# Two fused feed-forward layers on one core: every product and transpose cut to 64 rows, top and low half of the array as two streams

## The reference, cut to what matters

```
x   : 4 x 4096 x 192;  weight : 8 heads x 7 taps, softmaxed over the taps
a   = sum over k of w[head, k] * x[position - 6 + k]          (each head has 24 of the 192 columns)
h1  = a @ moe_w_in          (192 x 2048);   g1 = h1 * cos(h1)
y1  = g1 @ moe_w_out        (2048 x 192)
h2  = y1 @ moe2_w_in        (192 x 2048);   g2 = max(h2, 0)^2
out = g2 @ moe2_w_out       (2048 x 192)
```

## Time and profile before

| what | value |
|---|---|
| median of 3 runs | 2475.63 us (2473.64 to 2476.59) |
| the profiled execution's own time | 2478.0 us |
| its span | 2476.2 us |
| TensorE busy | 2409.9 us, 97% of the span, 10880 products and transposes |
| VectorE, ScalarE busy | 1869.2 us (75%), 1738.2 us (70%) |
| mean granted TensorE clock | 0.993 of full speed |
| transfers | 32.89 MB, 13 GB/s over the span |

### The profile page before, as it was taken

The page is one execution under the profiler, slowest core; times in us unless marked ns, Lnnn a source line. Parts: engine busy times, 40 slices in busy tenths (PEclk is TensorE's granted clock), DMA queues, the critical chain, the costliest instruction groups (busy, mean ns, idle before and its releaser), DMA issues.

```text
span 2476.2 us, 29392 instructions
## 1 busy us (share of the span) xinstructions
PE 2409.9 (97%) x10880; PEld 1994.4 (81%) x10880; DVE 1869.2 (75%) x2061; ACT 1738.2 (70%) x1805; POOL 24.8 (1%) x11
## 2 busy tenths in 40 slices
PE   4699999999999999999999999999999999999998
PEld 3488888888888888888888888888888888888886
DVE  7787777777777777777777777778777778777752
ACT  4577677767677767777767777776777776777774
POOL 1200000000000000000000000000000000000000
PEclk9899999999999999999999999999999999999998
DMA  3100000000000000000000000000000000000000
GB/s 108 39 1 13 14 9 10 13 6 13 13 6 13 13 6 13 13 6 13 8 11 13 13 6 13 6 13 13 13 6 13 6 13 13 13 6 6 7 7 13
DMA packets 39456, 32.89 MB, mean 13 GB/s; under 512 B 1676, under 2 KB 38668, under 8 KB 39180
## 3 DMA queue, kind: packets, MB, share of 16 engines
q1 hardware_dynamic: 39260, 32.61, 4.4%
q10 hardware_dynamic: 176, 0.00, 0.0%
HBM read 20.03 MB, written 12.58 MB: 13 GB/s over the span
## 4 chain that ended last, share of the span: by engine, by line
PE 94%; DVE 3%; ACT 2%; DMA 0%; issue 0%; SPq 0%; ACTq 0%
PE h L320 9%; PE h L321 9%; PE h L323 9%; PE h L322 9%; PE h L324 9%; PE y_B L340 5%; PE y_A L340 5%; PE y_B L341 5%; PE y_B L344 5%; PE y_B L342 5%; PE y_B L343 5%; PE y_A L342 5%; PE y_A L341 5%; PE y_A L343 5%; PE y_A L344 5%; PE h L366 1%
## 5 line engine op out<-in xcount | busy, mean ns | idle before, releaser
L554 DVE TENSOR_TENSOR g_lo<-g,g_hi 128x1024 fp32r<-128x1024 f32 x512 | 629.8, 1230 | 280.3 <-ACT g_hi L456 278.4
L456 ACT ACTIVATE g_hi<-g 128x1024 fp32r<-128x1024 f32 x512 | 538.0, 1051 | 50.0 <-DVE g L549 49.6
L446 ACT ACTIVATE w<-w,quarter 128x1024 f32<-128x1024 f32 x256 | 295.2, 1153 | 373.3 <-DVE w L542 373.3
L436 ACT ACTIVATE g<-h 128x1024 f32<-128x1024 f32 x256 | 261.2, 1020 | 199.6 <-PE h L324 199.5
L549 DVE TENSOR_TENSOR g<-w,g 128x1024 f32<-128x1024 f32 x256 | 316.0, 1234 | 60.1 <-ACT w L446 41.4
L542 DVE SCALAR_TENSOR_TENSOR w<-w,g 128x1024 f32<-128x1024 f32 x256 | 313.7, 1225 | 8.8
L540 DVE TENSOR_SCALAR w<-g 128x1024 f32<-128x1024 f32 x256 | 179.2, 700 | 147.8 <-ACT g L436 147.7
L438 ACT ACTIVATE g<-h 128x1024 f32<-128x1024 f32 x256 | 260.1, 1016 | 43.5 <-PE h L324 41.0
L440 ACT ACTIVATE g<-g 128x1024 f32<-128x1024 f32 x256 | 271.9, 1062 | 8.1
L340 PE MATMUL y_A<-g_hi,dn_lo_A 128*128 128x512 f32 x512 | 207.1, 405 | 24.4 <-DVE g_lo L554 24.4
L320 PE MATMUL h<-x_side_A,up_side_lo_A 128*128 128x512 f32 x512 | 200.5, 392 | 24.4 <-DVE x_side_A L589 20.5
(11 more groups left out here) (90 smaller groups left out, 4254.7 us busy)
## 6 DMA issues: line engine op xcount, KB each, us to landing
rows_in<-x SPq DMA_DIRECT2D x32, 384.0 KB, 3.3
out<-late SPq DMA_DIRECT2D x32, 384.0 KB, 2.6
late<-w_out SPq DMA_DIRECT2D x2, 1536.0 KB, 10.8
g<-w_in SPq DMA_DIRECT2D x1, 1024.0 KB, 5.7
g<-w_in SPq DMA_DIRECT2D x2, 512.0 KB, 8.6
late<-w_in SPq DMA_DIRECT2D x2, 512.0 KB, 4.4
late<-w_in SPq DMA_DIRECT2D x4, 256.0 KB, 5.5
taps<-weight ACTq DMA_DIRECT2D x4, 0.7 KB
```

What stands on the lines that cost most here:

```text
L446: act.activation(v, v, ACT.Sin, bias=quarter[:, 0:1], scale=-TURN).then_inc(cosine, 1)
L456: act.activation(g_hi[:, r, :, :], g[:, r, :, :], ACT.Copy).then_inc(hi_made[kind], 1)
L554: dve.tensor_tensor(g_lo[:, r, :, :], g[:, r, :, :], g_hi[:, r, :, :].bitcast(F32), ALU.subtract).then_inc(lo_made[kind], 1)
```

## The change

The array of 128 rows is used as two halves. Every product takes 64 rows of the stationary and of the moving operand: rows 0 to 63 (`top`) or 64 to 127 (`low`). TensorE's instructions alternate between the halves. In `up_and_down` the top half does the up projection of the slot (9 steps) and then its share of the down projection (10 steps), while the low half does the down projection first (10) and the up projection after it (9): 19 steps of one product on each half. Both halves add into the same bank, one after the other, and new semaphores (`up_top`, `down_top`, `down_low`, `turned_low`) keep them from being in one bank at once.

The side's low-by-high product needs 64 rows only. So an up projection has 4.5 products of 128 rows for a chunk in place of 5: 9 steps a half for the pair. For the odd chunk this needs the side's high part in the other 64 rows as well (`x_odd`), for the even chunk the weights (`up_even`); the copies to `x_odd` are one more ScalarE instruction for each tile of layer 1 and one more VectorE instruction for layer 2.

`LAG` becomes 4. Where the down projection's slot is X or Y there is none to pair with, and two up projections are joined with one down projection (`two_up_and_down`, 28 steps). X and Y slots pair transposes with a down projection (`turn_and_down`, 14 steps); a transpose is now of 64 rows, with a weight load of 128 columns and 64 moving columns, so there are twice as many. B0 moves from slot 2 to slot 3, and the splits of y_A and y_B move one slot later on ScalarE and VectorE. The halves of the output's side are added by ScalarE and VectorE (`y2_low`, `y2_summed`) where a product with the matrix `fold` did it.

```diff
-LAG = 3
-SLOTS = [("A", 0), ("A", 1), ("B", 0), ("A", 2), ("X", 0), ("B", 1), ("A", 3), ("B", 2), ("A", 4),
+LAG = 4
+SLOTS = [("A", 0), ("A", 1), ("A", 2), ("B", 0), ("X", 0), ("B", 1), ("A", 3), ("B", 2), ("A", 4),
          ("B", 3), ("A", 5), ("Y", 0), ("A", 6), ("B", 4), ("A", 7), ("B", 5), ("B", 6), ("B", 7)]
...
-            def up(turn, s, kind, p):
+
+
+            UP, DOWN = 4 * PAIR + 1, 5 * PAIR
+            SHORT = 2 * CB
+
+            def up_waits(turn, s, kind, p):
+                freed = turn.before(turn.slots, s, HB)
+                if freed:
+                    pe.wait_ge(taken[freed[0]], freed[1])
...
+                    pe.wait_ge(even_made, 2)
+
+            def up_step(turn, s, kind, p, rows, k):
+
+                even = 5 if rows is hi_rows[kind] else 4
+                n, j = (0, k) if k < even else (1, k - even)
+                if rows is low and j == 0:
+                    pe.wait_ge(up_top[kind][n], turn.count(kind, p))
+                f = slice((p * PAIR + n) * P, (p * PAIR + n + 1) * P)
+                dst = h[:, s % HB, n, :]
+                end = k in (even - 1, UP - 1)
+                z = rows is low and end
+                if j == 0:
+                    mm = pe.matmul(dst, up_side[kind][rows, f], xin_side[kind][rows, :], start=rows is top, stop=z)
+                if j == 1:
+                    mm = pe.matmul(dst, up_lo[kind][rows, f], xin_hi[kind][rows, :], start=False, stop=z)
+                if j == 2:
+                    mm = pe.matmul(dst, up_hi[kind][rows, f], xin_lo[kind][rows, :], start=False, stop=z)
+                if j == 3:
+                    mm = pe.matmul(dst, up_hi[kind][rows, f], xin_hi[kind][rows, :], start=False, stop=z)
+                if j == 4 and n == 0:
+                    mm = pe.matmul(dst, up_even[rows, p, :], xin_side[kind][rows, :], start=False, stop=z)
+                if j == 4 and n == 1:
+                    mm = pe.matmul(dst, up_side[kind][rows, f], xin_odd[rows, :], start=False, stop=z)
+                if rows is top and end:
+                    mm.then_inc(up_top[kind][n], 1)
+                if rows is low and k == UP - 1:
+                    mm.then_inc(filled[kind], 1)
+
...
                 if kind == "B" and p == 0 and turn.runs("Y"):
                     pe.wait_ge(y2_copied, turn.i - 1)
+                    pe.wait_ge(y2_summed, turn.i - 1)
                 pe.wait_ge(lo_made[kind], turn.count(kind, p, back))
+
+            def down_step(turn, r, kind, p, back, rows, k, first):
+
+                if k in (0, 6):
+                    other = (down_low if rows is top else down_top)[kind][k // 6]
+                    n = turn.count(kind, p, back) - (rows is first)
+                    if not isinstance(n, int) or n > 0:
+                        pe.wait_ge(other, n)
...
+                if m == 0 and j == 0:
+                    mm = pe.matmul(y[kind][:, 0, :], dn_lo[kind][rows, c, :], hi, start=a, stop=False)
...
+                if k in (5, DOWN - 1):
+                    mm.then_inc((down_top if rows is top else down_low)[kind][m], 1)
+
+            def up_and_down(turn, s, kind, p, down):
+
+                up_waits(turn, s, kind, p)
+                down_waits(turn, *down[1:])
+                for k in range(UP + DOWN):
+                    if k < UP:
+                        up_step(turn, s, kind, p, top, k)
+                    else:
+                        down_step(turn, *down, top, k - UP, low)
+                    if k < DOWN:
+                        down_step(turn, *down, low, k, low)
+                    else:
+                        up_step(turn, s, kind, p, low, k - DOWN)
+
+            def two_up_and_down(turn, s, kind, p, kind2, p2, down):
+
+                up_waits(turn, s, kind, p)
+                down_waits(turn, *down[1:])
+                for k in range(2 * UP + DOWN):
+                    if k == UP:
+                        up_waits(turn, s + 1, kind2, p2)
+                    if k < UP:
+                        up_step(turn, s, kind, p, top, k)
+                    elif k < 2 * UP:
+                        up_step(turn, s + 1, kind2, p2, top, k - UP)
+                    else:
+                        down_step(turn, *down, top, k - 2 * UP, low)
+                    if k < DOWN:
+                        down_step(turn, *down, low, k, low)
+                    elif k < DOWN + UP:
+                        up_step(turn, s, kind, p, low, k - DOWN)
+                    else:
+                        up_step(turn, s + 1, kind2, p2, low, k - DOWN - UP)
+
+            def turn_and_down(turn, s, kind, down):
+
+                down_waits(turn, *down[1:])
+                for k in range(DOWN + SHORT // 2):
+                    if k == 4:
+                        turn_waits(turn, s, kind)
+                    if k == DOWN - 1:
+                        pe.wait_ge(turned_low[kind], turn.count(kind, 0))
+                    if k < DOWN:
+                        down_step(turn, *down, top, k, top if k < 6 else low)
+                    else:
+                        turn_step(s, kind, top, 2 * (k - DOWN))
+                        turn_step(s, kind, top, 2 * (k - DOWN) + 1)
+                    if k < 4:
+                        down_step(turn, *down, low, 6 + k, low)
+                    elif k < 4 + SHORT // 2:
+                        for t in (2 * (k - 4), 2 * (k - 4) + 1):
+                            if kind == "X" or t < CB:
+                                turn_step(s, kind, low, t)
+                    else:
+                        down_step(turn, *down, low, k - 4 - SHORT // 2, top)
+
+            def up_alone(turn, s, kind, p):
+
+                up_waits(turn, s, kind, p)
+                for k in range(UP + 6):
+                    if k < UP:
+                        up_step(turn, s, kind, p, top, k)
+                    if k >= 6:
+                        up_step(turn, s, kind, p, low, k - 6)
+
...
+                    runs = turn.runs(kind)
+                    e, back, made, q = turn.earlier(s, LAG)
+                    down = made in "AB" and turn.runs(made, back) and (turn.ring(e, back) % RING, made, q, back)
+                    if kind in "AB" and runs and down:
+                        kind2, p2 = turn.slots()[s + 1] if s + 1 < NS else ("X", 0)
+                        _, back2, made2, _ = turn.earlier(s + 1, LAG)
+                        joined = kind2 in "AB" and turn.runs(kind2) and not (made2 in "AB" and turn.runs(made2, back2))
+                        if joined:
+                            two_up_and_down(turn, s, kind, p, kind2, p2, down)
                         else:
-                            up(turn, s, kind, p)
-                    e, back, kind, p = turn.earlier(s, LAG)
-                    if kind in "AB" and turn.runs(kind, back):
-                        down(turn, turn.ring(e, back) % RING, kind, p, back)
+                            up_and_down(turn, s, kind, p, down)
+                    elif kind in "AB" and runs:
+                        up_alone(turn, s, kind, p)
+                    elif runs and down:
+                        turn_and_down(turn, s, kind, down)
+                    elif runs:
+                        turn_alone(turn, s, kind)
+                    elif down:
+                        down_alone(turn, down)
...
-                    if s == 0 and turn.runs("A", 1):
-
-                        act.wait_ge(used["A"], turn.count("A", NP - 1, 1))
+                    if s == 1 and turn.runs("A", 1):
+
+                        act.wait_ge(down_low["A"][0], turn.count("A", NP - 1, 1))
+                        act.wait_ge(down_top["A"][1], turn.count("A", NP - 1, 1))
...
+                        act.activation(yt[top, 1, :], y["B"][low, 1, :], ACT.Copy).then_inc(y2_low, 1)
+                        act.activation(yt[:, 0, :], y["B"][:, 0, :], ACT.Copy).then_inc(y2_copied, 1)
...
                         act.activation(xin_side["A"][P - SIDE:P, :], conv_side[P - SIDE:P, :], ACT.Copy)
+                        act.activation(xin_odd[0:SIDE, :], conv_side[P - SIDE:P, :], ACT.Copy)
                         act.activation(xin_hi["A"][:, :], conv[:, :], ACT.Copy).then_inc(x1_hi, 1)
...
-                dve.tensor_copy(xin_side["B"][low, :], y_side[low, :]).then_inc(x2_step, 1)
+                dve.tensor_copy(xin_odd[SIDE:P, :], y_side[top, :])
+                dve.tensor_copy(xin_side["B"][top, :], y_side[top, :]).then_inc(x2_step, 1)
...
-                    if s == 0 and turn.runs("A", 1):
+                    if s == 1 and turn.runs("A", 1):
                         split_layer2(turn)
...
+                    if s == 4 and turn.runs("Y"):
+                        dve.wait_ge(y2_low, turn.i - 1)
+                        dve.tensor_tensor(yt[top, 1, :], y["B"][top, 1, :], yt[top, 1, :], ALU.add)\
+                           .then_inc(y2_summed, 1)
```

(46 more changed lines are left out.)

121 lines of the change are left out of this document (60 added, 61 removed).

## The result

The changed kernel takes 2568.63 us (median of 4, 2563.68 to 2572.67), the kernel before 2476.10 in the same comparison: a ratio of 1.0375, with a 95% interval from 1.0354 to 1.0396. The forecast was 2513: slower was right, but the forecast had 37 us more where 93 were measured. The profiled execution took 2572.67 us.

A forecast was written before the change was run, and what follows sets the result against it. TensorE's work was taken as the bound. A turn of 72.1 + 2.0 + 1.6 = 75.7 us is 1.0 more, times 31 turns +31, ends +6: 2478.0 becomes 2515 profiled, 2513 against the runs; range 2430 to 2600.

The forecast's parts named there:

- The step: One product on either half takes 0.2267 us: each half keeps the whole array's pace and the weight loads just fit.
- The bare columns: Rival: a step takes only its 512 columns, 0.2133 us; 73.3 us a turn, about 2436 us; chance 0.24.
- the stolen columns: Rival: two weight loads take 27 ns from the stream, step 0.240 us; 78.2 us a turn, 2590 us; chance 0.14.
- load and product in series: Rival: a half's weight load and product follow each other, 0.335 us a step; about 3400 us; chance 0.08.
- halves in series: Rival: the two halves don't run at once, 0.453 us a step; about 4550 us; chance 0.05.
- TensorE's work: Per turn, 312 steps at 0.2267 us make 70.7, plus 1.4 for doubled transposes: 72.1 us.
- The wait before A0: TensorE waits 2.0 us a turn for x1_made before A0, including 0.63 for the copy to x_odd.
- The wait before B1: TensorE waits 1.6 us a turn for B0's buffer, behind the split of y_A; part perhaps already at B0.
- The turn: Work of 72.1 plus waits of 2.0 and 1.6 make 75.7 us, 1.0 more than 74.68.
- the waits don't bind: Rival: ScalarE and VectorE catch up where they idle now; 72.1 us a turn, 2402 us; chance 0.07.
- the last sentence on the clock: The clock could fall, but waits of 2 us between stretches of 15 should not do that; no term in the sum.
- The ends: Program start and end: extra steps from LAG 4 and unpaired projections, between 0 and 12 us, taken as 6.

The follow-up runs named there:

- ten: The kernel called both, with the dropped half product put back as lo x lo, 10 steps a half in each up projection instead of 9: 2485.7 us.
- xlate: Changed kernel with layer 1's copy to x_odd moved behind g_hi of A7 in slot 16, out of the chain to x1_made: 2501.2 us.
- yfirst: Changed kernel with ScalarE in slot 1 copying y_A before A0's sine instead of behind it: 2505.6 us.
- filler: Changed kernel with 8 more steps (16 products of 64 rows) on TensorE before the wait for A0's input: 2552.4 us.
- split14: Changed kernel with the last tap moved from slot 15 to 14 and the mixed input's split from slots 15/16 to 14/15: 2484.6 us.
- both: Changed kernel with the edits of split14 and yfirst together: 2404.2 us.
- before_late: Kernel before the change, full-array products, with five more 64-row copies on ScalarE before x_hi_A: 2594.1 us.
- dose: The kernel called yfirst, with the last two taps of the mixing in slot 13: 2439.3 us.

## Why the prediction was right and where it was wrong

- **The step, 0.2267 taken: right.** In a slot without a wait the 19 steps take 4.31 us (L390 at 1190.07, and again at 1194.38 at the same place of the next slot), 0.2267 each; right behind a wait they are a little longer (7 steps from 1201.82 to 1203.42, 0.2286 each). The bare columns (0.2133), the stolen columns (0.240), load and product in series (0.335) and halves in series (0.453) are all out. The Trainium skill, "TensorE: Matmul & The Clock Gate", Part 3, has it that a load overlaps a running product only of other rows; the timeline shows loads that start with the product before them on the same half (1202.06 beside 1202.05). Its 4 ns for each further tile, which gave 0.231, don't show in the slots without a wait.
- **TensorE's work, 72.1 us a turn: 1.4 too high.** The term that was too large is the 1.4 us for transposes: in ten, where TensorE never waits, they cost nothing, and 312 steps of 0.2267 are 70.7.
- **The wait before A0, 2.0: measured 2.05** (2.28 us on the low half from B7's last product at 254.81 to A0's first at 257.09, less a step). **Its 0.63 for x_odd: measured 0.65** (75.57 - 74.92, xlate).
- **The wait before B1, 1.6 "part of it perhaps already at B0": measured 0.70 + 1.57.** The chain was right, as yfirst shows; the size was short by 0.7.
- **The turn, 75.7: measured 75.6 where the clock holds, and part of that is luck.** All that comes on top of the 70.7 is 4.9, not 3.6: the three waits are 4.3, and behind each the first step takes 0.31 to 0.34 in place of 0.23 (257.00 to 257.34), which the sum left out; 0.3 us of the 4.9 I can't place. Work 1.4 too high and waits 1.3 too low cancel. The rival "the waits don't bind" is out.
- **VectorE near 77% busy: measured 75.6%** from 200 to 1200 us (755.64 of 1000), since the turns are longer than was forecast.
- **The step that failed is the last sentence on the clock:** "waits of 2 us between stretches of 15 should not do that". They do: 33 times in the loop, 1.6 us each, 52 of 93 us, for which the sum had no term. Rows 2 were no ground for that sentence, since a stretch with TensorE 61% busy at 0.80 says nothing on how short an idle time suffices. That idle time brings it is shown by filler (work in its place), split14, yfirst and both (wait gone, its slow stretches gone) and before_late (the same in full-array products). Which of the waits of 1.4 and 1.8 us are followed by a slow stretch stays open.
- **The ends, 6 of 0 to 12: measured 9.7 + 7.9 = 17.6,** over the bound. A bound by steps alone (12 us) left out the clock and the waits. Up to the fourth tile the mean granted clock is 0.91 where it was 0.94; from the last tile on TensorE is idle for 18.0 us where it was 13.2. How the 17.6 divide further was not tested.

## What to carry to other kernels

Two row-tiled streams keep the full pace of the array on each half, weight loads included, so a product of 192 rows can cost 1.5 full ones instead of 2; that gain (2.5 us a turn) is real, and the streams alone give next to nothing. Interleaving two pieces of work nearly doubles the time from the first product of each to its result (here from 10 x 0.2267 = 2.3 us to 19 steps, 4.3 us), so every consumer chain that had slack has to be counted again, instruction by instruction, and reordered before the gain shows. A wait of TensorE of 1.4 to 2.4 us can cost 1.6 us more behind it by the clock: read the granted clock of the stretch behind each wait, and shorten or fill the wait.

## What the runs showed of the hardware that I had not expected

- After 1.4 to 2.4 us of idle TensorE between stretches of dense products the granted clock fell to the level of 1.2 GHz (0.50, 0.51) for 3.4 us in many turns, with 64-row and 128-row products alike: after 2.35 us in 21 of 28 turns (before_late), after 1.8 us in 19 (changed) and 26 (yfirst), after 1.4 us in 2 to 14. After 1.2 us or less it never did in the loops of these kernels (0 of 28 in xlate, none in dose). In the turn shown of the changed kernel it fell 0.8 us after products had begun again; in the one of before_late the first product after the wait ran slow already (0.50 from 1197.50 on).
- Two products of 64 rows on the two halves start 0.00 to 0.15 us apart in the changed kernel, and both run at the pace of a whole-array product.
- Three weight loads in a step, where transposes stand beside a product, cost no time that a turn shows (ten: 74.33 us, and 328 steps of 0.2267 are 74.36).
